# Weight work of the second layer moved from GpSimd to VectorE, and the output chunks regrouped

## The reference

```
x   = attention(q, k, v)                    # 2304 x 512
h   = x @ w_in;  r = relu(h);  g = s*r*r + b
x   = g @ w_out                             # first layer
h   = x @ w2_in; g = h - tanh(h)
out = g @ w2_out                            # second layer
```

## Time and profile before

| | us |
|---|---|
| median of 3 runs (908.51 to 908.93) | 908.61 |
| the profiled execution | 906.39 |
| its span, first to last instruction | 904.2 |
| PE busy in it | 879.7 (97%) |
| DVE busy | 586.6 (65%) |
| ACT busy | 471.9 (52%) |
| POOL busy | 416.3 (46%) |
| mean granted clock of PE | 0.994 of full speed |

### The profile page before, as it was taken

One profiled execution on the slowest core, in us unless ns is written; L12 is line 12 of the kernel. 1 busy time (PEld: TensorE's weight loads), 2 busy tenths in 40 slices (PEclk: granted clock), 3 DMA queues, 4 the chain that ended last, 5 costly groups with the idle time before them and its releaser, 6 DMA issues.

```text
span 904.2 us, 15887 instructions
## 1 busy us (share of the span) xinstructions
PE 879.7 (97%) x5956; PEld 823.2 (91%) x5956; DVE 586.6 (65%) x759; ACT 471.9 (52%) x1128; POOL 416.3 (46%) x372
## 2 busy tenths in 40 slices
PE   7999999999999999999999878999999999999998
PEld 6889999999999999999999767989889888989887
DVE  5658599989999999982201587454844447543444
ACT  3899585467546755445656434334543336433332
POOL 6568474966497653525726653213431125212110
PEclk9999999999999999999999989999999999999999
DMA  8972453353344123102103321101420101401012
GB/s 216 276 240 55 126 145 85 89 128 86 97 114 104 58 59 80 35 2 96 36 28 94 110 92 32 39 24 47 140 70 24 47 24 26 115 24 47 24 47 71
DMA packets 57903, 73.56 MB, mean 81 GB/s; under 512 B 19110, under 2 KB 36068, under 8 KB 57828
## 3 DMA queue, kind: packets, MB, share of 16 engines
q1 hardware_dynamic: 56233, 72.12, 28.8%
q10 hardware_dynamic: 1595, 0.43, 0.2%
HBM read 63.10 MB, written 9.44 MB: 80 GB/s over the span
## 4 chain that ended last, share of the span: by engine, by line
PE 92%; DVE 4%; ACT 2%; issue 1%; DMA 1%; SPq 1%; ACTq 0%; DVEq 0%
PE acc L2197 23%; PE hid L2169 22%; PE hid L2234 19%; PE acc L2251 14%; PE pa L2251 7%; PE pa L2127 1%; PE pa L2094 1%; DMA dkey<-in_k_dram 1%; PE pa L1969 1%; PE pa L2111 1%; DVE sum L1628 1%; PE pa L2140 1%; DVE wq_raw L1576 1%; DVE g2l L1633 0%; PE acc L1961 0%
## 5 line engine op out<-in xcount | busy, mean ns | idle before, releaser
L1233 POOL TENSOR_TENSOR gl<-relu,gh 128x288 fp32r<-128x288 f32 x128 | 129.5, 1016 | 155.2 <-PE acc L2197 109.8
L1249 POOL TENSOR_TENSOR w2bl<-w2b_raw,w2bh 128x512 fp32r<-128x512 f32 x48 | 62.4, 1320 | 213.4 <-ACT w2bh L1890 213.4
L2197 PE MATMUL acc<-gh,wbh 128*128 128x288 f32 (+1 forms) x512 | 154.5, 302 | 0.0
L2169 PE MATMUL hid<-xh,wah 128*128 128x288 f32 x512 | 153.5, 301 | 0.3 <-ACT relu L1859 0.2
L2197 PE MATMUL acc<-gl,wbh 128*128 128x288 f32 (+1 forms) x512 | 151.5, 296 | 0.0
L2197 PE MATMUL acc<-gh,wbl 128*128 128x288 f32 (+1 forms) x512 | 151.2, 295 | 0.0
L2169 PE MATMUL hid<-xh,wal 128*128 128x288 f32 x512 | 150.4, 295 | 0.0
L2169 PE MATMUL hid<-xl,wah 128*128 128x288 f32 x484 | 142.0, 294 | 0.0
L2234 PE MATMUL hid<-x2h,wqh 128*128 128x384 f32 x336 | 113.4, 337 | 11.5 <-DVE sum L1613 4.9
L1859 ACT ACTIVATE relu<-hid 128x288 f32<-128x288 f32 x128 | 52.3, 408 | 130.6 <-PE hid L2169 109.8
L2234 PE MATMUL hid<-x2l,wqh 128*128 128x384 f32 x336 | 113.5, 338 | 0.0
(11 more groups left out here) (209 smaller groups left out, 1884.6 us busy)
## 6 DMA issues: line engine op xcount, KB each, us to landing
w2b_raw<-in_moe_w_out_dram SPq DMA_DIRECT2D x24, 512.0 KB, 3.7
kl<-in_k_dram SPq DMA_DIRECT2D x23, 240.0 KB
vl<-in_v_dram SPq DMA_DIRECT2D x23, 240.0 KB
x2T<-ystage SPq DMA_DIRECT2D x8, 576.0 KB, 3.2
own<-in_q_dram SPq DMA_DIRECT2D x11, 384.0 KB
wa_raw<-in_moe_w_in_dram SPq DMA_DIRECT2D x4, 1024.0 KB, 8.6
wb_raw<-in_moe_w_out_dram SPq DMA_DIRECT2D x4, 1024.0 KB, 10.2
x2raw<-x2T SPq DMA_DIRECT2D x10, 384.0 KB, 3.9
```

The costliest lines, as they stand in the source:

```text
L1233: g.tensor_tensor(out=gl[:, turn % LRING1, 0:NS], in0=relu[:, f % 2, :], in1=gh[:, turn % GRING1, 0:NS].bitcast(F32), op=ALU.subtract).the ...
L1249: g.tensor_tensor(out=w2bl[:, slot, :], in0=w2b_raw[:, slot, :], in1=w2bh[:, slot, :].bitcast(F32), op=ALU.subtract).then_inc(s_w2bl, 1)
L2169: one = pe.matmul(dst, w[:, group, d, cols], x[:, j % XRING, d, :], start=i == 0, stop=i == 3 * KT - 1)
L2197: one = pe.matmul(acc[:, d, n], w[:, f, cols], g[:, turn % ring, n], start=(f == 0 and p == 0), stop=(f == FT - 1 and p == 2))
```

## The change

In words:

- `w2a_low` goes from POOL to DVE, and it and `w2a_high` are done in three parts, matrices 0 to 2, 3 to 4 and 5 to 6. `w2_sums` of quarter q waits in the plan for `u2` of pair q-2.
- `w2b_low` of the first eight pairs goes from POOL to DVE, as two steps; from pair 8 on it stays on POOL.
- The order of products and chunks: p6 before p1; chunks in twos, behind p1, p7 and p5, from pair 2 on. Pairs 0, 1 and the last have orders of their own.
- The last `finish1` is four steps in the plan, one for each bank, and each chunk of pair 0 waits for its bank alone.
- `t1` of the second and third tile waits in the plan and by a semaphore for p1 of the third pair before that tile.

The diff, cut to its core:

```diff
+W2PARTS = [(0, 3), (3, 5), (5, 7)]
+EARLY2 = 3
...
-        o.add("DVE", 1.8, (2, q), ("w2_sums", q), [("load_w2a", q)])
-        o.add("ACT", 1.65, (2, q), ("w2a_high", q), [("w2_sums", q)])
-        o.add("POOL", 4.7, (2, q), ("w2a_low", q), [("w2a_high", q)])
+        paced = [("u2", q - 2)] if q > 1 else []
+        o.add("DVE", 1.8, (2, q), ("w2_sums", q), [("load_w2a", q)] + paced)
+        for part, (m0, m1) in enumerate(W2PARTS):
+            o.add("ACT", 0.2 + 0.22 * (m1 - m0), (2, q), ("w2a_high", q, part), [("w2_sums", q)])
+            o.add("DVE", 0.17 + 0.26 * (m1 - m0), (2, q), ("w2a_low", q, part), [("w2a_high", q, part)])
...
-        o.add("POOL", 2.9, (2, n), ("w2b_low", n), [("w2b_high", n)])
+        if n < QUADS:
+            for f in range(2):
+                o.add("DVE", 0.7, (2, n), ("w2b_low", n, f), [("w2b_high", n)])
+        else:
+            o.add("POOL", 2.9, (2, n), ("w2b_low", n), [("w2b_high", n)])
...
+            if j:
+                before.append(("product", QUADS * j - EARLY2, "p1"))
...
-        order = ["p1", outs[0], "p6", outs[1], "p2", "p7", outs[2], "p4", outs[3], "p5", outs[4], "p3", outs[5]]
+        order = (["p6", "p1", outs[0], "p2", "p7", outs[1], "p4", "p5", outs[2], "p3"] if n == 0 else
+                 ["p6", "p1", outs[0], outs[1], "p2", outs[2], "p7", outs[3], "p4", "p5", outs[4], "p3", outs[5]] if n == 1 else
+                 ["p6", "p1", outs[0], outs[1], "p2", "p7", outs[2], outs[3], "p4", "p5", outs[4], outs[5], "p3"])
         if n == TILES2 * QUADS - 1:
+            order = ["p6", "p1", outs[0], outs[1], "p2", "p7", outs[2], "p4", "p5", outs[3], "p3", outs[4], outs[5]]
             order += [("out2", n, i) for i in range(BLOCK2)]
...
-                    o.add("ACT", 1.9, (0,), ("finish1", last), [chain, ("store1", last - 1)])
-                    o.add("SP", 0.6, (0, last), ("store1", last), [("finish1", last)], kbytes=600)
+                    for d in range(KT):
+                        o.add("ACT", 0.48, (1,) if d else (0,), ("finish1", last, d), [chain, ("store1", last - 1)])
+                    o.add("SP", 0.6, (0, last), ("store1", last), [("finish1", last, KT - 1)], kbytes=600)
...
+                if j:
+                    g.wait_ge(s_product["p1"], QUADS * j - EARLY2 + 1)
...
+            elif kind == "w2a_low":
+                q, part = key
+                mats = slice(*W2PARTS[part])
+                ve.wait_ge(s_w2ah, len(W2PARTS) * q + part + 1)
+                ve.tensor_tensor(wql[q][:, mats, :, :], wq_raw[q][:, mats, :, :], wqh[q][:, mats, :, :].bitcast(F32),
+                                 ALU.subtract).then_inc(s_w2al, 1)
...
-                    pe.wait_ge(s_w2al, q + 1)
+                    pe.wait_ge(s_w2al, len(W2PARTS) * (q + 1))
...
-                    pe.wait_ge(s_y, KT * TILES1)
+                    pe.wait_ge(s_y, KT * (TILES1 - 1) + min(i, KT - 1) + 1)
```

More of the change, by code:

```diff
@@ L529, in plan @@
                 if j == 0:
-                    after.append(("w2a_low", q))
+                    after.append(("w2a_low", q, len(W2PARTS) - 1))
                 if q == 0:
@@ L543, in plan @@
                 one, i = step[1:]
-                after = [chain, ("w2b_low", one)] + [("g2_low", one, m) for m in ((0, 1) if i < BLOCK2 // 2 else (2, 3))]
+                after = [chain, ("w2b_low", one, 1) if one < QUADS else ("w2b_low", one)] + [("g2_low", one, m) for m in ((0, 1) if i < BLOCK2 // 2 else (2, 3))]
                 if one % QUADS == 0:
-                    after.append(("finish2", one // QUADS - 1, i) if one else ("finish1", last))
+                    after.append(("finish2", one // QUADS - 1, i) if one else ("finish1", last, min(i, KT - 1)))
                 o.add("PE", 1.37, (1,), step, after)
@@ L1235, in gpsimd_program @@
                                 ).then_inc(s_gl, 1)
[L1238 to L1242, removed]
             elif kind == "w2b_low":
                 n, = key
+                if n == QUADS:
+                    g.wait_ge(s_w2bl, 2 * n)
                 for f in range(2):
@@ L1578, in vector_program @@
                 ve.tensor_tensor(raw[:, S4, :, :], raw[:, A12, :, :], raw[:, S2, :, :], ALU.subtract).then_inc(s_w2sum, 1)
+            elif kind == "w2a_low":
[4 more added lines that the diff above has]
+                                 ALU.subtract).then_inc(s_w2al, 1)
+            elif kind == "w2b_low":
+                n, f = key
+                slot = n % 2 * 2 + f
+                ve.wait_ge(s_w2bh, 2 * n + f + 1)
+                ve.tensor_tensor(w2bl[:, slot, :], w2b_raw[:, slot, :], w2bh[:, slot, :].bitcast(F32), ALU.subtract
+                                 ).then_inc(s_w2bl, 1)
             elif kind == "x2_low":
@@ L1867, in scalar_program @@
             elif kind == "finish1":
-                j, = key
+                j, *banks = key
                 sc.wait_ge(s_used, FT * (j + 1))
+                banks = banks or range(KT)
                 if j == 0:
@@ L1875, in scalar_program @@
                     sc.wait_ge(s_stored, 16 * j)
-                for d in range(KT):
+                for d in banks:
                     sc.activation(ystage[:, d, :], acc[:, d, 0:NS], ACT.Identity, bias=bias[:, d:d + 1],
@@ L1880, in scalar_program @@
             elif kind == "w2a_high":
-                i, = key
+                i, part = key
+                mats = slice(*W2PARTS[part])
                 sc.wait_ge(s_w2sum, 4 * (i + 1))
-                sc.activation(wqh[i][:, :, :, :], wq_raw[i][:, :, :, :], ACT.Copy).then_inc(s_w2ah, 1)
+                sc.activation(wqh[i][:, mats, :, :], wq_raw[i][:, mats, :, :], ACT.Copy).then_inc(s_w2ah, 1)
             elif kind == "w2b_high":
```

## The result

| us | before | after |
|---|---|---|
| median of the runs | 908.59 (4 runs, 908.51 to 908.93) | 892.44 (4 runs, 891.94 to 892.53) |
| the profiled execution | 906.39 | 892.53 |
| its span | 904.2 | 890.7 |

The ratio is 0.982, 95% interval 0.9803 to 0.9837: 16.2 us less by the medians, 13.9 by the profiled executions. Beside the later experiments the kernel before ran 905.3 to 909.1 us, with medians of 907.1 to 907.8, and the changed kernel once more 892.76: ratio 0.9838 (0.9824 to 0.9853), 14.7 us. The profiled execution of before was thus a low one of its scatter; what makes the scatter was not found.

What follows compares the result with a forecast made beforehand. PE bounds steady pairs; pairs 0 to 2 wait on DVE, held by POOL. Profiled 906.4 -14.6 -1.3 +0.6 = 891.1; from the median, 908.6-15.3 = 893.3 us, range 890.5 to 896 (0.62), 8 in 10 889.5 to 899.

Steps and rivals of the forecast that it cites:

- What bounds it, and why DVE is late: PE bounds steady pairs; in pairs 0 to 2 POOL's w2a_low, some 4.1 us, holds DVE operations with two SBUF inputs.
- The 16.1 us lost in pairs 0 to 2: 59.5 us against 43.4 undisturbed: 11.4 of PE waits, some 3.2 of half clock, 1.5 of restarts.
- Part 1: Moving w2a_low from POOL to DVE in three parts recovers most of the first pairs' loss: -14.6 us, clock included.
- The 0.5 us a pair for pairs 0 and 1: Waits expected to remain where outputs stand singly; with 0.5 for the rest, 1.5 us left over in all.
- Part 2: Chunks in twos save 0.06 us in each of 22 pairs: -1.3 us.
- The lower bound: For chunks in twos: 0 gained, if the second chunk of two gains nothing when a product follows it.
- What the order gives away: Before the next pair's p1, c12 has p6 (1.04 us) as cover, not a chunk (1.39); 0.15 us spare, cost 0.
- Part 3: At the two changes of tile, c12 has less room and may be late: +0.3 us each, +0.6 in all.
- A: Rival: weight work on DVE delays critical sums, c12 above all, in six to seven pairs; 903 us, chance 0.16.
- B: Rival: c12 late in all 22 pairs, POOL's w2b_low holding the operation ahead from pair 8; 912 us, chance 0.05.
- C: Rival: everything hidden, no leftover at the start or changes of tile, 0.09 us a pair; 889.7 us, chance 0.12.
- D: Rival: waits move to ACT or a load, and half of the 16 us stay; 901 us, chance 0.05.

Runs made afterwards that it cites:

- pool_reads: Changed kernel plus six useless POOL operations of 128x1024 that read SBUF in pairs 0 to 2; 897.05 us.
- pool_writes: Changed kernel plus fifteen useless POOL memsets of 128x1024, which write SBUF and read none, in pairs 0 to 2; 893.03 us.
- old_order: Changed kernel with the earlier kernel's order of products and chunks in every pair; 894.56 us.
- parts_on_pool: Changed kernel with w2a_low, still in three parts, on POOL in place of DVE; 892.67 us.
- order_alone: Kernel before with only the new order of products and chunks, weight work staying on POOL; 912.83 us.
- unpaced: Changed kernel without the spacing: w2_sums no longer waits for u2 of two pairs before; 892.29 us.
- parts_alone: Kernel before with w2a_high and w2a_low in three parts, w2a_low still on POOL, old order, no spacing; 902.68 us.

## Why the prediction was right

893.3 was forecast, 892.44 measured, the kernel 15.3 us faster by the one and 16.2 by the other. By its steps:

- **What bounds it, and why DVE is late.** Right for the holds, and shown by `pool_reads` and `pool_writes`.
- **The 16.1 us lost in pairs 0 to 2.** Right in size: 59.5 became 43.4 us. But the prediction puts all of it down to the holds. `old_order`, which has the new weight work and no hold in pairs 0 to 2, took 45.8: 13.7 us came back with the weight work, and the other 2.4, nearly all in pair 0, with the order.
- **Part 1, -14.6.** -13.7 by `old_order`; -16.1 with the order's cover in pair 0, which the prediction counts here. The 0.5 us a pair for pairs 0 and 1 did not come, nor the 0.5 for the rest. That the engine is what frees DVE was too narrow: `parts_on_pool` does the same.
- **Part 2, -1.3.** Wrong: 0. The step that failed is the price of a pair of chunks, read from the earlier trace rows, where chunks are followed by chunks; where a product stands behind them, that product takes 1.06 in place of 1.04. The lower bound held. The Trainium skill, "TensorE: Matmul & The Clock Gate", by whose spacing the order is worth nothing, came out right on that sum; its spacing did not: it gives 216 ns for 512 columns, and the chunks here ran 227 to 232. What the order does bring is cover, which the prediction put at nothing: 2 us beside the new weight work, against 5 us lost beside the old (`order_alone`, 912.8 against 907.4).
- **What the order gives away.** Right in place and size: steady pairs show p1 starting 0.01 to 0.03 us late at most, and c12 is what is late where an operation is held before it.
- **Part 3, +0.6.** Right in place, too small: +2.05. I priced half a hold of 1.3 us; at pair 16 a dif of 1.48 us and an x2_low of 1.45 us, each held by POOL's x2_low, stood before c12:

```profile
750.23 1.48 DVE L1655 TENSOR_TENSOR sum<-sum,tanh 128x384 f32<-128x384 f32 x1
751.63 1.45 DVE L1610 TENSOR_TENSOR x2l<-ostage,x2h 128x384 fp32r<-128x384 f32 x1
753.01 0.54 DVE L1646 TENSOR_TENSOR odd<-hid,odd 128x384 f32<-128x384 f32 x1
```

The three errors cancel in part: -1.5, +1.3 and +1.45 make +1.25. That the forecast lies within 0.9 us of the median is partly luck. The sum against the profiled execution (891.1 forecast, 892.5 measured) is off by more than the one against the median, since the median of before stood 2.2 above its profile.

- **Rivals.** A (DVE late) did not occur in pairs 0 to 7, not even unpaced. B's place, c12 behind a held operation, was seen at two pairs of 22, with x2_low in w2b_low's stead. C came nearest in pairs 0 to 2 and was wrong on the rest. D fell: no load and no ACT row took the waits. (The load of w2_out lands 3.7 us after its issue by the page of the kernel before, not 3.9; nothing hung on it.)

## What to carry to other kernels

Where a DVE operation lasts far longer than its like, lay POOL's rows beside it before thinking of DVE's own load: a long POOL operation that reads SBUF stopped DVE's operations with two SBUF inputs until it ended, and everything queued on DVE behind them. Cutting it shorter than the spare time of the waits behind it was worth as much as moving it in the new order (`parts_on_pool`), and much less in the old (`parts_alone`). Before putting a loss down to contention, ask what the order would cost with every engine free: pair 0 lost some 2 us by its list alone. Price an order of matmuls from a place with the same neighbours on both sides; and count what each reordering takes from the one wait with the least cover, at the stretch where that engine is busiest.

## What the runs showed of the hardware

The hold works both ways. Of the six useless POOL operations of `pool_reads`, the two that began with no DVE operation with two SBUF inputs in progress took 1.90 us; the four that began during one took 2.09, 2.09, 2.22 and 2.67. The spacing of equal matmuls depends on their neighbours: 0.227 us for 128x512 among their like, 0.232 in a chunk between products.
